# One attention-to-experts kernel: a swizzled slot table that is loaded whole once, routing moved up one batch step, weight loads spread over five chunks

## The reference

```python
# 1. linear attention, 4 batches, 8 heads, 768 steps, head size 48
for t in range(S):
    cur = einsum('bhd,bhe->bhde', u * k_t, v_t)
    y[:, :, t] = einsum('bhd,bhde->bhe', r_t, state + cur)
    state = w * state + einsum('bhd,bhe->bhde', k_t, v_t)
# 2. mixture of 8 experts, one per token, with a skip test
do_compute = x @ w_skip > 0
e_idx = argmax(x @ w_gate); gate = softmax(x @ w_gate)[e_idx]
out = x;  out[do_compute] += gate * (relu(x @ w1[e_idx]) @ w2[e_idx])
# 3. dense
h = x @ w_in;  out = (h * clip(h + 3, 0, 6) / 6) @ w_out      # 384 -> 2048 -> 384
```

## Time and profile before

| | |
|---|---|
| median of 3 runs | 783.18 us (781.2 to 785.65) |
| the profiled execution | 784.61 us, span 782.4 us |
| TensorE busy | 719.6 us (92%) |
| VectorE, ScalarE, GpSimd busy | 49%, 34%, 18% |
| HBM read, written | 53.71 MB, 12.80 MB |
| mean granted clock of TensorE | 0.969 |

### The profile page before, as it was taken

One profiled execution on the slowest core, in us unless ns is written; L12 is line 12 of the kernel. 1 busy time (PEld: TensorE's weight loads), 2 busy tenths in 40 slices (PEclk: granted clock), 3 DMA queues, 4 the chain that ended last, 5 costly groups with the idle time before them and its releaser, 6 DMA issues.

```text
span 782.4 us, 13231 instructions
## 1 busy us (share of the span) xinstructions
PE 719.6 (92%) x5021; PEld 660.9 (84%) x5021; DVE 382.7 (49%) x705; ACT 267.8 (34%) x508; POOL 142.9 (18%) x186
## 2 busy tenths in 40 slices
PE   4999999990899899994999999999999999999997
PEld 3998978880799898994889999989998998989986
DVE  5676666563577657653544433343333334334332
ACT  1222222223555555532434333233332323323222
POOL 6456546644322222210000000000000000000000
PEclk9999999995799999996999999999999999999999
DMA  8578999802165645513000200020020001001001
GB/s 142 123 172 166 228 230 192 201 31 66 55 230 195 203 145 202 188 66 97 1 0 1 81 1 1 8 73 1 1 81 0 1 21 61 0 1 41 1 1 40
DMA packets 106853, 65.54 MB, mean 84 GB/s; under 512 B 81346, under 2 KB 101092, under 8 KB 106800
## 3 DMA queue, kind: packets, MB, share of 16 engines
q1 hardware_dynamic: 103040, 59.99, 29.0%
q0 software_dynamic: 2816, 4.60, 1.7%
q10 hardware_dynamic: 944, 0.21, 0.2%
HBM read 53.71 MB, written 12.80 MB: 85 GB/s over the span
## 4 chain that ended last, share of the span: by engine, by line
PE 76%; DMA 9%; issue 6%; POOL 5%; DVE 2%; POOLq 0%; ACT 0%; DVEq 0%; SPq 0%; ACTq 0%
PE bank L775 9%; PE bank L774 9%; PE bank L773 9%; PE bank_Y L773 6%; PE bank_Y L775 6%; PE bank_A L774 6%; PE bank_A L775 6%; PE bank_Y L774 6%; PE bank_A L773 6%; DMA xg<-x_scratch,who 5%; PE bank_Y L744 3%; PE bank_A L708 2%; POOL slot_scratch L420 2%; PE bank_Y L734 2%; DMA who<-slot_scratch 2%
## 5 line engine op out<-in xcount | busy, mean ns | idle before, releaser
L1143 DVE TENSOR_TENSOR g_lo<-g,g_hi 128x512 fp32r<-128x512 f32 x96 | 66.4, 692 | 67.0 <-ACT g_hi L613 67.0
L1141 DVE SCALAR_TENSOR_TENSOR g<-cut,bank_A 128x512 f32<-128x512 f32 x60 | 41.2, 687 | 95.7 <-ACT cut L610 95.7
L613 ACT ACTIVATE g_hi<-g 128x512 fp32r<-128x512 f32 x96 | 60.7, 632 | 72.7 <-DVE g L1141 72.7
L775 PE MATMUL bank_A<-mT_hi,wi_lo 128*128 128x512 f32 x180 | 71.0, 394 | 0.0
L610 ACT ACTIVATE cut<-bank_A 128x512 f32<-128x512 f32 x60 | 35.9, 598 | 102.3 <-PE bank_A L775 101.7
L774 PE MATMUL bank_A<-mT_lo,wi_hi 128*128 128x512 f32 x180 | 70.9, 394 | 0.0
L773 PE MATMUL bank_A<-mT_hi,wi_hi 128*128 128x512 f32 x180 | 70.1, 389 | 0.0
L773 PE MATMUL bank_Y<-wo_hi,g_hi 128*128 128x384 f32 x192 | 66.2, 345 | 0.0
L775 PE MATMUL bank_Y<-wo_hi,g_lo 128*128 128x384 f32 x192 | 65.1, 339 | 0.0
L774 PE MATMUL bank_Y<-wo_lo,g_hi 128*128 128x384 f32 x192 | 64.7, 337 | 0.0
L775 PE MATMUL bank<-wo_hi,g_lo 128*128 128x384 f32 x192 | 64.1, 334 | 0.0
(11 more groups left out here) (182 smaller groups left out, 1615.0 us busy)
## 6 DMA issues: line engine op xcount, KB each, us to landing
raw<-in_moe_w_dram SPq DMA_DIRECT2D x24, 512.0 KB, 5.7
raw<-in_moe_w_dram SPq DMA_DIRECT2D x8, 1536.0 KB, 6.9
r_in<-in_r_dram SPq DMA_DIRECT2D x24, 192.0 KB, 4.2
k_in<-in_k_dram SPq DMA_DIRECT2D x24, 192.0 KB, 4.3
v_in<-in_v_dram SPq DMA_DIRECT2D x24, 192.0 KB, 5.1
x_scratch<-y_sb SPq DMA_DIRECT2D x24, 192.0 KB, 4.7
out_dram<-o_sb SPq DMA_DIRECT2D x12, 384.0 KB, 2.8
m_in<-x_scratch SPq DMA_DIRECT2D x5, 768.0 KB, 5.3
```

The source lines that it names most:

```text
L613: eng.activation(g_hi[f % 4][:, :], g[f % 2][:, :], ACT.Copy).then_inc(s_ghi, 1)
L775: return eng.matmul(dst, a_lo, b_hi, start=False, stop=stop)
L1141: eng.scalar_tensor_tensor(g[f % 2][:, :], cut[f % 2][:, :], 1.0, p_H[f % 3][:, :], ALU.min, ALU.mult).then_inc(s_g, 1)
L1143: eng.tensor_tensor(g_lo[f % 4][:, :], g[f % 2][:, :], g_hi[f % 4][:, :].bitcast(F32), ALU.subtract).then_inc(s_glo, 1)
```

## The change

Four things change together.

1. *The table's order.* Slot s = 128 col + p is stored at row 192 p + col, where it was at row s. VectorE works this out with three more small operations per group. The whole table then lies in SBUF by one load, `who_all`, with slots of a tile in two neighbouring columns. Only the first tile's slots are loaded apart. For later tiles GpSimd reads the tile's column number from `plan_col` and copies two columns; SyncE has no slot loads left in its stream. Expert 1's w1 waits for the first tile's gathers.
2. *Routing one batch step up.* The running sums are made in step 1, `count` and the slot numbers in step 2.
3. *The last chunk's groups* are three batches and one (`LATE = 3`); the per-batch logits stand elsewhere in TensorE's order.
4. *Weight loads.* w_in in eight pieces over chunks 1 and 2, expert 0's w1 in chunk 3 as before, its w2 in four pieces in chunk 4, w_out in three pieces in chunk 5.

```diff
@@ -38,11 +38,13 @@
 
 ROUND = (4, 8, 12)
 SHIFT = 4
-RT_SHIFTED, RT_CHOICE, RT_SUMS, RT_TOTAL, RT_PICKED, RT_ALL = 3, 7, 8, 12, 13, 15
-C_WIN, C_WOUT, C_EXP = 1, 2, 3
-W_PARTS = B
+RT_SHIFTED, RT_CHOICE, RT_SUMS, RT_TOTAL, RT_PICKED, RT_ALL = 3, 7, 8, 12, 13, 18
+C_WIN, C_W1, C_W2 = (1, 2), 3, 4
+WI_PARTS, W2_PARTS = 2 * B, B
+WO_ROWS = (0, 6, 11, 16)
 POOL_LO = 8
 SETS = 3
+LATE = 3
 GW = 32
 N_TOK = 8
 N_PAR = 3
...
@@ -306,39 +313,37 @@
                     store(b, c)
                     if c < NC - 1:
                         load(b, c + 1)
-                    if c == C_WIN:
-                        own = slice(b * F2 // W_PARTS, (b + 1) * F2 // W_PARTS)
+                    if c in C_WIN:
+                        part = C_WIN.index(c) * B + b
+                        own = slice(part * F2 // WI_PARTS, (part + 1) * F2 // WI_PARTS)
                         eng.dma_start(wi_raw[:, :, own], wi_dram[:, :, own]).then_inc(s_wi, 16)
-                    if c == C_WOUT:
-                        own = slice(b * G2 // W_PARTS, (b + 1) * G2 // W_PARTS)
+                    if c == C_W1 and b < KC:
+                        eng.dma_start(raw1[:, b, :], w1[0, b * P:(b + 1) * P, :]).then_inc(s_raw1[b], 16)
+                    if c == C_W2:
+                        own = slice(b * G1 // W2_PARTS, (b + 1) * G1 // W2_PARTS)
+                        eng.dma_start(raw2[:, own, :], w2[0].rearrange("(g p) n -> p g n", p=P)[:, own, :]).then_inc(s_raw2, 16)
+                    if c == NC - 1 and b < len(WO_ROWS) - 1:
+                        own = slice(WO_ROWS[b], WO_ROWS[b + 1])
                         eng.dma_start(wo_raw[:, own, :], wo_dram[:, own, :]).then_inc(s_wo, 16)
-                    if c == C_EXP and b < KC:
-                        eng.dma_start(raw1[:, b, :], w1[0, b * P:(b + 1) * P, :]).then_inc(s_raw1[b], 16)
-                    if c == C_EXP and b == KC:
-                        eng.dma_start(raw2[:, :, :], w2[0].rearrange("(g p) n -> p g n", p=P)).then_inc(s_raw2, 16)
             for done in s_slots:
                 eng.wait_ge(done, 16 * B * NC // SETS)
-            eng.dma_start(who[0][:, :, :], slot_dram[0:TT, :].rearrange("(t p) two -> p t two", p=P)).then_inc(s_who[0], 16)
+            eng.dma_start(who[0][:, :, :], slots_by_p[:, 0:TH, :]).then_inc(s_who0, 16)
+            eng.dma_start(who_all[:, :, :], slots_by_p).then_inc(s_who_all, 16)
             n_tiles = tiles_planned(eng)
-
-            def next_slots(j, m, i):
-                with eng.If(n_tiles > j + 1):
-                    row = eng.value_load(plan_row[0:1, bass.ds(j + 1, 1)], min_val=0, max_val=SLOTS - TT)
-                    wait(eng, s_y2ev, TH * j)
-                    wait(eng, s_ids, j)
-                    eng.dma_start(who[1 - i][:, :, :], slot_dram[bass.ds(row, TT), :].rearrange("(t p) two -> p t two", p=P)).then_inc(s_who[1 - i], 16)
 
             def experts(j, m, i):
                 if isinstance(j, int) and j == 0:
-                    return next_slots(j, m, i)
+                    return
                 with eng.If(n_tiles > j):
                     e = eng.value_load(plan[0:1, bass.ds(j, 1)], min_val=0, max_val=E - 1)
                     wait(eng, s_w1lo, KC * j)
+                    if isinstance(j, int) and j == 1:
+                        for done in s_xg[0]:
+                            eng.wait_ge(done, 16)
                     for kc in range(KC):
                         eng.dma_start(raw1[:, kc, :], w1[bass.ds(e, 1), kc * P:(kc + 1) * P, :].rearrange("a p f -> p (a f)")).then_inc(s_raw1[kc], 16)
                     wait(eng, s_w2lo, G1 * j)
                     eng.dma_start(raw2[:, :, :], w2[bass.ds(e, 1), :, :].rearrange("a (g p) n -> p (a g) n", p=P)).then_inc(s_raw2, 16)
-                next_slots(j, m, i)
 
             expert_loop(eng, experts)
 
@@ -442,8 +447,8 @@
                         scatters(c - 2, c - 2, range(b * 2, b * 2 + 2))
                 identify(c)
             scatters(NC - 2, NC - 2, range(B))
-            scatters(NC - 1, NC - 1, range(0, B // 2))
-            scatters(NC, NC - 1, range(B // 2, B))
+            scatters(NC - 1, NC - 1, range(0, LATE))
+            scatters(NC, NC - 1, range(LATE, B))
 
             def fetch(i):
 
@@ -455,15 +460,19 @@
             eng.wait_ge(s_tok, N_TOK + 1)
             for b in range(B):
                 eng.wait_ge(s_st[b], 16 * NC)
-            eng.wait_ge(s_who[0], 16)
+            eng.wait_ge(s_who0, 16)
             fetch(0)
             n_tiles = tiles_planned(eng)
 
             def gather(j, m, i):
 
-                eng.wait_ge(s_who[i], 16 * (m + 1))
+                if isinstance(j, int) and j == 1:
+                    eng.wait_ge(s_who_all, 16)
+                col = eng.value_load(plan_col[0:1, bass.ds(j, 1)], min_val=0, max_val=E * EC - TH)
+                wait(eng, s_y2ev, TH * (j - 1))
                 eng.sem_inc(s_pass, 1)
-                wait(eng, s_y2ev, TH * (j - 1))
+                eng.tensor_copy(who[i][:, :, :], who_all[:, bass.ds(col, TH), :]).then_inc(s_who, 1)
+                wait(eng, s_who, j)
                 eng.sem_inc(s_pass, 1)
                 fetch(i)
 
...
@@ -682,9 +691,7 @@
             def logits_direct(b):
 
                 eng.wait_ge(s_Xev, B * (NC - 1) + b + 1)
-                if b == 0:
-                    eng.wait_ge(s_rt, routed(NC - 2, RT_CHOICE))
-                if b == 2:
+                if b == B - 1:
                     eng.wait_ge(s_rt, routed(NC - 1, RT_CHOICE))
                 for kc in range(KC):
                     t = eng.matmul(p_logit1[:, b, 0:E + 1], xT[:, kc, b, :], gate_w[:, kc, 0:E + 1], start=kc == 0, stop=kc == KC - 1)
@@ -714,10 +721,12 @@
                         logits_back(c - 1)
                     if b == 2 and c:
                         eng.wait_ge(s_rt, routed(c - 1, RT_CHOICE))
+                        count(c - 1, p_count, 0, B, 1)
                     if b == 3 and c:
-                        count(c - 1, p_count, 0, B, 1)
-                    if b == 0 and c > 1:
-                        eng.wait_ge(s_rt, routed(c - 2, RT_PICKED))
+                        eng.wait_ge(s_rt, routed(c - 1, RT_PICKED))
+                    if b == 3 and c == NC - 1:
+                        for done in range(LATE - 1):
+                            logits_direct(done)
                     x_transposes((b - 1) % B, c - (b == 0))
                 if n < NT - 1:
                     transposes((b + 1) % B, c + (b + 1) // B)
@@ -736,6 +745,8 @@
                 m.then_inc(s_Yst, 1)
                 if b == 0 and c:
                     logits(c - 1)
+                if n == NT - 1:
+                    logits_direct(2)
 
                 eng.wait_ge(s_Aev, n + 1)
                 for q in range(NPAIR):
@@ -744,8 +755,6 @@
                         m = eng.matmul(p_Y[:, o, 2 * q * HD:2 * (q + 1) * HD], A_sb[i][:, o, q, :], v_in[b][:, h * HD:(h + 2) * HD],
                                        start=False, stop=h == H - 1, skip_group_check=True)
                 m.then_inc(s_Y, 1)
-                if c == NC - 1 and b:
-                    logits_direct(b - 1)
 
             def products(b):
 
@@ -763,11 +772,10 @@
                 for b in range(B):
                     step(b, c)
             eng.wait_ge(s_Xev, NT - 1)
-            eng.wait_ge(s_rt, routed(NC - 2, RT_PICKED))
+            count(NC - 1, p_countA, 0, LATE, 0)
             x_transposes(B - 1, NC - 1)
-            count(NC - 1, p_countA, 0, B // 2, 0)
             logits_direct(B - 1)
-            count(NC, p_countB, B // 2, B, 1)
+            count(NC, p_countB, LATE, B, 1)
 
             def three(dst, a_hi, a_lo, b_hi, b_lo, start, stop):
                 eng.matmul(dst, a_hi, b_hi, start=start, stop=False)
...
@@ -1018,12 +1026,15 @@
                 rt(eng.tensor_tensor(pick[:, some, :], p_ranks[:, some, :], chosen[:, some, :], ALU.mult))
                 assert rt.count[0] == RT_PICKED
                 rt(eng.tensor_reduce(slot_f[:, some], pick[:, some, :], AXX, ALU.add))
-                rt(eng.tensor_tensor(slots[c % SETS][:, some], slot_f[:, some], miss[:, some], ALU.add))
+                rt(eng.tensor_tensor(slot_i[:, some], slot_f[:, some], miss[:, some], ALU.add))
+                rt(eng.tensor_scalar(slot_p[:, some], slot_i[:, some], P - 1, None, ALU.bitwise_and), free=True)
+                rt(eng.tensor_scalar(slot_c[:, some], slot_i[:, some], LOG_P, None, ALU.logical_shift_right))
+                rt(eng.scalar_tensor_tensor(slots[c % SETS][:, some], slot_p[:, some], float(E * EC), slot_c[:, some], ALU.mult, ALU.add))
                 eng.sem_inc(s_slot, 1)
                 assert rt.count[0] == RT_ALL
 
             every = slice(0, B)
-            half_A, half_B = slice(0, B // 2), slice(B // 2, B)
+            half_A, half_B = slice(0, LATE), slice(LATE, B)
             rts = [steps_of(group) for group in range(NC + 1)]
 
             def routing(b, c):
@@ -1033,15 +1044,15 @@
```

(32 more changed lines are left out.)

2 lines of the change are left out of this document (1 added, 1 removed).

## The result

The changed kernel takes 760.58 us (median of 4 runs, 759.62 to 761.11), the kernel before 783.84 on the same chip (4 runs, 781.2 to 785.65): a ratio of 0.970, 95% interval 0.967 to 0.974. The forecast was 760.5. The profiled execution took 760.35 us, its span is 758.6, against 784.61 and 782.4.

What follows compares the result with a forecast made beforehand. TensorE, busy 92% of the span, bounds the kernel; only its standstills before 356 us can be won. 6.2 + 3.9 + 3.5 + 7.9 + 1.7 = 23.2 us off 784.61 gives 761.4, 760.5 predicted; range 754 to 771.

Steps and rivals of the forecast that it cites:

- Attention, 6.2 forecast: Chunks 2 to 4: weights over five chunks and routing one step up win 6.2 of the 6.4 us of stalls.
- the stalls are the weights': Attention: weight loads raise the DMA share to 0.96 and cause the stalls; spread, all DMA stalls go, bounds 0 and 6.4.
- routing one step up is covered: Attention, step 2: VectorE's added 1.2 us fits its 1.25 us idle before bank_Y; uncovered, it would cost at most 1.2.
- One sign of the prediction: Attention: if right, GpSimd has no wait for slots within chunks 2 to 4.
- Slot scatters, 3.9 forecast: Between attention and the first tile: last slot scatter lands at 183.4 instead of 187.3, gain 3.9 us.
- The queue of 2.08 us each: Last chunk's slot scatters: landings stay 2.08 us apart, taken as the nearest row, giving the gain of 3.9.
- an upper bound, 5.7: Last chunk's slot scatters: if the spaced addresses end the queue, the last lands at 181.6, gain 5.7 us.
- First gather, 3.5 forecast: Before the first tile: expert 1's weights wait for both gathers, so the second takes 3.3 us, not 6.85; gain 3.5.
- Tiles, 7.9 + 1.7 forecast: Expert tiles: earlier w1 ends 8.5 us of waits for rows, 0.1 a tile left (7.9); no clock drop in one (1.7).
- the gather's own time: Rival, gathers: they take 6 us even without weights beside them, so moving weights gives nothing; 776 us, chance 0.12.
- The rival on attention: Rival, attention: the stalls are not the weights', SyncE's queue may be full, so 6.2 us stays; 766 us, chance 0.06.
- The slow GpSimd rival: Rival, tiles: GpSimd's column read and copy cost 6 us a tile in place of 0.7; 791 us, chance 0.04.

Runs made afterwards that it cites:

- wi later: The changed kernel with the last four of GpSimd's eight wi_lo pieces moved behind VectorE's split of tile 1's w1, ahead of the first result's scatter: 760.35 us.
- the split behind: The changed kernel with VectorE's split of expert 0's w1 held until GpSimd has issued both first gathers: 761.28 us.
- the second try: The changed kernel, but SyncE issues w1 of tile j (from 2 on) only when GpSimd has copied tile j's slots: 779.46 us, ratio to before 0.988.

## Why the prediction was right, and where it was only lucky

The time was right within 0.1 us, which is luck: terms were off on both sides. By the two traces, 23.8 us of span:

*Attention, 6.2 forecast.* 6.4 measured, at 0.79 of DMA time from chunk 2 on, forecast 0.66 to 0.75. The step from there to "the stalls are the weights'" is half wrong. The weights alone end most of the stalls (5.1), but spaced addresses with routing one step up end them as well (5.9), and on top of those the weights bring nothing. By these traces the stalls needed both a heavy load and slow slot writes; how slow slot writes hold up the loads of r, k and v, no run shows. That the addresses bear on attention I had not seen at all, though the row was there: scatters landing in 6.4 us in chunk 1. That routing one step up is covered held with these addresses (TensorE's busy time in chunks 2 to 4 is full). One sign of the prediction did not come: GpSimd still waits 9.2 us for slots in chunks 2 to 4, in three places, and it costs nothing, since TensorE never stands.

*Slot scatters, 3.9 forecast.* 38.36 us from chunk 5's mask to the last landing became 32.33, 6.0. The queue of 2.08 us each, which I kept as the nearest row, is gone: it was the case that I had as an upper bound, 5.7. The same code in seven other traces takes 33.3 to 34.7, a gain of 3.6 to 5.1. The trace behind the 6.0 is thus the best of eight. The clock tells some of these apart. Windows of the changed kernel, and of wi later, whose attention is the same code:

```profile
162.00:166.00 4.00, 3.99 (x43) 3.80 (x42) 1.83 (x11) 1.01 (x3) 1.96 (x2) 1.00 0.63 216
```

```profile
162.00:166.00 4.00, 4.00 (x36) 3.94 (x34) 0.78 (x5) 0.71 (x2) 1.82 (x2) 0.75 0.57 195
```

The clock is the last column but two. In the first it is still 1.00, and the span to the landing is 32.33; in the second it has already fallen from 2.4 towards 1.2 GHz and the span is 34.7. The last logits and counts run at whichever is granted.

*First gather, 3.5 forecast.* 2.7 measured, but not by the step I named. I had the gather at 3.3 us and it took 3.85, 0.9 of it GpSimd's longer issue; with the split held back it takes 3.1. (At 2.45 us a gather, the prediction's first gather term is 4.4 and not 4.2.) The wait that was to protect it brought nothing (the run without it).

*First tile, nothing forecast.* 1.8 lost. I checked that ScalarE's work was covered, and not what GpSimd's eight pieces, which move with the gather, would fall on. Before, they ended at 203.05, ahead of VectorE's first w2_lo at 203.90; now they ended at 192.72 and w2_lo was due at 188.83. By the Trainium skill (SBUF — State Buffer, Who interferes with whom) a VectorE instruction with two SBUF inputs contends with a GpSimd instruction that reads SBUF, by an exclusive lock; the trace agrees, and adds that w2_lo waited through some four of GpSimd's operations in a row. That rule would have named this loss, and with four of the pieces moved away 2.1 us of it came back (34.3 to 32.2). The same section infers that VectorE's tensor_tensor doesn't stall GpSimd's making of descriptors; here a gather's issue takes 1.8 to 1.9 us beside one and 1.0 to 1.1 without, in the changed kernel and the run with the split behind, so for this gather, which also takes its row numbers from SBUF, the measurement decides against it.

*Tiles, 7.9 + 1.7 forecast.* 11.2 measured. The gather starts 3.8 us behind the scaling, forecast 4.2, and lands in 2.8 to 3.4 us, forecast 3.3. w1 is issued 3.6 us ahead of the scaling at 224.76, where I had said some 6. That it is still nearly through when the gather starts at 228.59 is luck: it moves at 306 GB/s where I had taken 238, and 9 x 306 = 2.75 of the 3.15 MB are moved from 218 to 227.

```profile
218.00:227.00 9.00, 9.00 (x60) 9.00 (x59) 5.78 (x9) 3.05 (x7) 1.77 (x2) 1.00 0.95 306
```

Of the 11.2, 8.5 is idle time (of the 117.41 us TensorE was busy 108.87, of the 106.17 now 106.15), so the 0.1 us a tile that I left did not come. The other 2.7 is busy time: 1.5 in the tile where the clock fell (19.37 to 17.82), forecast 1.7, and 1.2 in the other five, forecast at nothing; why those matmuls were longer stays open.

*The dense part, nothing forecast.* From the barrier's end at 359.0 and at 334.4 to the end of the span, 0.8 us longer (423.4 to 424.2) with the same code. The windows, of the kernel before and of the changed one, show why:

```profile
359.00:372.00 13.00, 7.23 (x22) 5.58 (x23) 5.72 (x11) 1.57 (x3) 0.00 (x0) 0.50 0.41 123
```

```profile
347.40:349.40 2.00, 2.00 (x7) 1.57 (x6) 0.69 (x1) 1.14 (x3) 0.00 (x0) 0.58 0.00 0
```

In both, TensorE stands at the barrier ahead of this part and then begins its products at 1.2 GHz. Before, it begins them at 367.83 and has 2.4 GHz from 372.04 on, 4.2 us later; now it begins at 343.27 and has it from 349.18 on, 5.9 us later. These 1.7 us more at half speed are worth some 0.8, an estimate from these rows.

Of the rivals, the gather's own time falls with the second try (779 in place of 762, gathers of 6.3 to 6.7 us). By the Trainium skill (DMA: Bandwidth & Descriptors, Queues, rings and completion order) an engine takes turns between its queues, packet by packet. From that the prediction inferred that a gather is little hurt by a weight load, which the page does not say; here the gather's time doubles. The rival on attention falls with the stalls gone, but it had a part of the truth: the weights alone weren't what made them. The slow GpSimd rival falls with the row of the copy: 0.19 us, and 0.89 from there to the gather. (Against it the prediction says that the trace disagrees with the page's 6 us. It does not: that figure in the Trainium skill, GPSIMD Engine Reference, 2.1 Instruction dispatch, is for the first call of a freshly loaded kernel, and not for each turn.)

## What to carry to other kernels

Before blaming a bandwidth, look at what small writes cost on the same DMA engines: here the addresses alone were worth as much as spreading the weight loads alone (ratios 0.990 and 0.989). A prefetch should be through, not merely issued, when a gather starts on which the next step waits; a lead of 0.7 us in place of 7.2 to 8.3 cost 17.5 us. And when a step moves earlier, list what moves with it on the engines whose operations slow each other, not only on those that wait.
